# Channel mix down product: one 512-column instruction for two products of the high part, half sums added by VectorE

## The reference, cut to what matters

```python
def _moe2_ref(x, mu_k, mu_r, w_k, w_v, w_r):
    x_prev = np.concatenate([np.zeros((B, 1, D)), x[:, :-1, :]], axis=1)
    xk = mu_k * x + (1.0 - mu_k) * x_prev
    xr = mu_r * x + (1.0 - mu_r) * x_prev
    k = np.maximum(xk @ w_k, 0.0)          # 256 -> 1024
    v = k * k @ w_v                        # 1024 -> 256: the down product
    r = 1.0 / (1.0 + np.exp(-(xr @ w_r)))  # the gate
    return r * v
```

## Time and profile before

| | us |
|---|---|
| median of 3 runs | 1606.61 (1606.55 to 1608.92) |
| the profiled execution, its own time | 1606.98 |
| its span in the profile | 1605.1 |

### The profile page before, as it was taken

The page is one execution under the profiler, slowest core; times in us unless marked ns, Lnnn a source line. Parts: engine busy times, 40 slices in busy tenths (PEclk is TensorE's granted clock), DMA queues, the critical chain, the costliest instruction groups (busy, mean ns, idle before and its releaser), DMA issues.

```text
span 1605.1 us, 30457 instructions
## 1 busy us (share of the span) xinstructions
PE 1505.6 (94%) x11046; PEld 1435.8 (89%) x11046; DVE 1035.9 (65%) x1665; ACT 896.1 (56%) x1709; POOL 340.2 (21%) x375
## 2 busy tenths in 40 slices
PE   6988856699999999999999978999999999999998
PEld 6878736699999999999999977999999999999998
DVE  4766679666666566666666636767676666767574
ACT  1553436476566566665665635656565555556563
POOL 2331227373333333333333310000000000000000
PEclk9998977799999999999999998999999999999999
DMA  8054211665565665665655510110101010101010
GB/s 230 1 158 144 93 79 54 247 241 214 206 234 197 209 240 198 223 224 199 230 216 199 221 39 29 38 52 27 52 26 52 26 52 26 52 26 52 26 40 27
DMA packets 56248, 196.84 MB, mean 123 GB/s; under 512 B 13942, under 2 KB 40326, under 8 KB 46984
## 3 DMA queue, kind: packets, MB, share of 16 engines
q1 hardware_dynamic: 45640, 171.02, 30.5%
q0 software_dynamic: 10560, 25.24, 4.9%
HBM read 160.27 MB, written 39.64 MB: 125 GB/s over the span
## 4 chain that ended last, share of the span: by engine, by line
PE 88%; DVE 5%; issue 3%; POOL 1%; DMA 1%; ACT 1%; SPq 0%; DVEq 0%; POOLq 0%; ACTq 0%
PE ps L603 77%; PE ps L531 3%; PE ps L562 2%; PE ps L611 2%; PE ps L660 1%; PE ps L551 1%; DVE hot_blk L1058 1%; PE ps L552 1%; DVE zv L979 1%; DMA xg<-rows,idx 0%; ACT d L729 0%; DMA tau_b<-tau 0%; DVE cum L1018 0%; ACT square L757 0%; DVE k2f L1151 0%
## 5 line engine op out<-in xcount | busy, mean ns | idle before, releaser
L603 PE MATMUL ps<-we,ht 128*128 128x256 f32 x2640 | 329.7, 284 | 0.0
L603 PE MATMUL ps<-xgt,we 128*128 128x256 f32 x2640 | 327.8, 284 | 1.4 <-DVE xgt L1087 1.4
L603 PEld LDWEIGHTS ps<-xgt,we 128*128 128x128 f32 x2640 | 322.7, 193 | 1.8 <-DVE xgt L1087 1.8
L603 PEld LDWEIGHTS ps<-we,ht 128*128 128x128 f32 x2640 | 319.8, 192 | 0.0
L1098 DVE SCALAR_TENSOR_TENSOR ht<-ps,ht 128x512 fp32r<-128x512 f32 x220 | 146.2, 684 | 217.4 <-ACT ht L789 217.2
L603 PE MATMUL ps<-w_split,k_split 128*128 128x256 f32 x2304 | 280.5, 283 | 0.2 <-DVE k_split L1144 0.2
L603 PEld LDWEIGHTS ps<-w_split,k_split 128*128 128x128 f32 x2304 | 278.2, 192 | 0.4 <-DVE k_split L1144 0.4
L603 PE MATMUL ps<-x_split,w_split 128*128 128x512 f32 x1152 | 268.0, 392 | 6.1 <-DVE x_split L1139 6.1
L1093 DVE TENSOR_TENSOR we<-we_raw,we 128x1024 fp32r<-128x1024 f32 x220 | 263.3, 1218 | 13.5 <-ACT we L779 13.4
L603 PEld LDWEIGHTS ps<-x_split,w_split 128*128 128x128 f32 x1152 | 216.1, 189 | 50.7 <-DVE x_split L1139 6.5
L859 ACT ACTIVATE relu<-ps 128x512 f32<-128x512 f32 x192 | 115.0, 599 | 214.8 <-PE ps L603 214.8
(11 more groups left out here) (142 smaller groups left out, 1423.7 us busy)
## 6 DMA issues: line engine op xcount, KB each, us to landing
we_raw<-w_e SPq DMA_DIRECT2D x55, 2048.0 KB, 8.2
rows<-xr SPq DMA_DIRECT2D x4, 3084.0 KB, 9.4
xin<-x SPq DMA_DIRECT2D x16, 768.0 KB, 12.9
xm<-moe SPq DMA_DIRECT2D x24, 512.0 KB, 4.0
out<-yc SPq DMA_DIRECT2D x24, 512.0 KB, 3.2
xg<-rows,idx POOLq DMA_INDIRECT x110, 4.8
moe<-yo,idx_out POOLq DMA_INDIRECT x110, 5.2
f<-c_f SPq DMA_DIRECT2D x1, 1664.0 KB, 17.0
```

Source lines behind the costliest of these rows:

```text
L603: ins = mm(o, a(i), b_(k), start=first_ and n == 0, stop=last_ and n == 2)
```

## The change

Two edits belong together.

On TensorE, the high part of `k_split` is the stationary operand of two products, with the high and with the low part of `w_v`. They become one instruction of 512 columns, whose moving operand is the view `wv2` over both parts: the left half of a bank takes high by high, the right half high by low. The third product, low by high, is added to the left half. So a group of 128 tokens fills one bank alone; groups 0 and 2 share bank 6, and groups 1 and 3 bank 7, one after the other.

On VectorE, each group is read by a `tensor_reduce` that adds the two halves of its bank into `vsum[j]`, in SBUF, and counts `c_vs`; a multiplication by `sig` of that group follows one group later. `c_v` now counts groups instead of tiles, and TensorE waits on `c_vs` before it starts a group: before j=2 for the reduction of j=0 of the same tile, before j=3 for that of j=1, and before j=0 and j=1 for those of the tile before.

```diff
+        vsum = [part(f"vsum{n}", [D]) for n in range(J)]
...
+        wv2 = w_split[:, :, DC * F:DC * F + FC * D].rearrange("p k (c d) -> p k c d", c=FC)
...
                 pe.wait_ge(c_kl, (t + 1) * FC)
-                wait(pe, c_y, t)
                 for j in range(J):
+                    wait(pe, c_vs, t * J + (j - 1))
+                    bank = ps[:, 6 + j % 2, :]
                     for f in range(FC):
-                        last = mm3(ps[:, 6 + j // 2, (j % 2) * D:(j % 2 + 1) * D],
-                                   lambda i: k_split[:, i, f, j * P:(j + 1) * P],
-                                   lambda k: wv[k][:, f, :], f == 0, f == FC - 1)
-                last.then_inc(c_v, 1)
+                        mm(bank.rearrange("p (k d) -> p k d", k=2), k_split[:, 0, f, j * P:(j + 1) * P], wv2[:, :, f, :],
+                           start=(f == 0), stop=False)
+                        last = mm(bank[:, 0:D], k_split[:, 1, f, j * P:(j + 1) * P], wv[0][:, f, :],
+                                  start=False, stop=(f == FC - 1))
+                    last.then_inc(c_v, 1)
...
                 if f == 0:
-                    wait(act, c_v, t)
+                    wait(act, c_v, t * J)
...
-                dve.wait_ge(c_v, t + 1)
                 dve.wait_ge(c_sig, t + 1)
                 wait(dve, c_out[s], t // 2 * 16)
-                v.tensor_tensor(yc[s].rearrange("p (n j) d -> p n (j d)", n=2), ps[:, 6:8, :],
-                                sig.rearrange("p (n j) d -> p n (j d)", n=2), ALU.mult).then_inc(c_y, 1)
+
+                def gated(j):
+                    dve.wait_ge(c_vs, t * J + (j + 1))
+                    return v.tensor_tensor(yc[s][:, j, :], vsum[j], sig[:, j, :], ALU.mult)
+
+                for j in range(J):
+                    dve.wait_ge(c_v, t * J + (j + 1))
+                    v.tensor_reduce(vsum[j], ps[:, 6 + j % 2, :].rearrange("p (k d) -> p d k", k=2), AX.X, ALU.add
+                                    ).then_inc(c_vs, 1)
+                    if j:
+                        gated(j - 1)
+                gated(J - 1).then_inc(c_y, 1)
```

More of the change, by code:

```diff
@@ L342, in fft_moe_channel_mix @@
         c_sig = sem("c_sig")
+        c_vs = sem("c_vs")
         c_y = sem("c_y")
```

## The result

Five runs of the changed kernel have a median of 1642.1 us (1640.95 to 1644.46), against 1607.95 us (1606.55 to 1608.92) for five of the kernel before on the same chip: a ratio of 1.0218, 95% interval 1.0204 to 1.0232, so 34 us slower. The prediction was 1649 us, with 1637 to 1684 as its range. The profiled execution took 1644.46 us with a span of 1642.6.

A forecast was written before the change was run, and what follows sets the result against it. TensorE's unbroken stream was taken to bound the channel mix at 26.18 us a tile. 23 tiles x 1.81 us plus 0.21 for the last make 41.8; 1606.61 + 41.8 = 1648.4, given as 1649 us, range 1637 to 1684.

The forecast's parts named there:

- The bound and the place: Channel mix: TensorE alone bounds it; a new wait ahead of j=2 stalls 2.22 us, 1.81 us more per tile.
- the 6.6 that was given as a sign of being wrong: Prediction is wrong if VectorE starts the first reduction before 6.6 us into the down product.
- The pair at 347.3 ns: Down product: one 512-column plus one 256-column matmul take 347.3 ns, bounds 334.6 and 360 ns.
- The forecast saving of 0.41 us a tile: Down product: 32 pairs take 11.11 us instead of 11.52, saving 0.41 us of TensorE time a tile.
- The reduction at 1.02 us: VectorE's new strided reduction of 512 PSUM elements takes 1.02 us, with 0.68 and 1.97 us as ends.
- the low end (0.68): VectorE's reduction priced like a plain copy of 512 elements out of PSUM, 0.68 us; whole kernel then 1640 us.
- its 23 equal tiles: The sum counts 23 tiles at 1.81 us more each, all but the last tile.
- Release and restart, 0.15: After VectorE's reduction of j=0, TensorE loses 0.04 us for the release and 0.11 us for the restart.
- VectorE after the last group, covered: VectorE's 1.85 us behind the down product's end just fit the 2.04 us before the first k2f.
- The clock rival: Stalls in the channel mix also drop TensorE's clock: 1.70 us each, 1688 us if all 23, 1668 if half; chance 0.30.
- The argument for holding off: Against a clock fall: first-stage waits had 96- and 146-column instructions around them; here 256 and 512 columns run back to back.
- Nearly free wide instructions: Down product: a 512-column matmul takes 120 ns like a narrow one, so not slower, about 1605.5 us; chance 0.05.

The follow-up runs named there:

- the run with the steps: Changed kernel plus 22 VectorE instructions behind its last result, reading PSUM and SBUF at various steps; only durations read; 1659.41 us in one run.
- The run with 248 elements more: Changed kernel plus a short extra reduction of 248 elements ahead of that of j=0 in each tile; 1662.27 us, ratio 1.0354.

## Why the prediction was right

**The bound and the place.** Right: 23 waits, all ahead of the third group, each tile longer by the wait less what the second half saves. The wait alone put into the kernel before gives 0.99 us of it. Each reduction more adds 0.60 us to the wait (1.46, 2.06, 2.66), and the second half saves 0.17: 1.42 of the 1.45 us that the changed kernel shows. The trace has the reduction start 6.53 us into the down product, just under the 6.6 that was given as a sign of being wrong; its record begins 0.07 us ahead of the end of the subtraction's, which is at 6.60.

**The pair at 347.3 ns.** 353 in a full stream, 346 behind a wait (1330.58 to 1335.43 holds 14 pairs), inside the bounds. The forecast saving of 0.41 us a tile is really 0.22 once the wait is gone.

**The reduction at 1.02 us.** This is the step that was off: 0.689 us, the low end (0.68) that the prediction carried. It read L979 as a dear PSUM operand, and the run with the steps shows that its dear operand is the one in SBUF; L1041 is SBUF as well. With 0.68 the prediction's own sum gives 1640 us, the runs 1642.1; its 23 equal tiles leave out the first tile's 2.7 us on top, 1.1 for the sigmoid and 1.6 for the clock. The estimate of 0.66 us from the Trainium skill, VectorE: DVE Perf Modes, section "The TRN2 errata", was the better guide; the trace's 0.689 is 4% over it.

**Release and restart, 0.15.** Right: 0.04 from the reduction to TensorE, and the first pair behind the wait takes 0.46 us where the next ones take 0.35.

**VectorE after the last group, covered.** Right: the first k2f still finds VectorE idle, for 0.83 us in the changed kernel as against 0.82.

**The clock rival.** It happened once, in the first tile behind 2.59 us, and at none of the 22 waits of 1.46 us; at the 1.8 us that the priced reduction makes it happens in a third of the tiles. The run with 248 elements more is the kernel that the prediction summed to 1649 us, and it takes 1662. So the sum with 1.02 us lacked a term, and that the measured 1642 came out nearer to it is luck: the reduction was cheaper, and the clock stayed up with it. The argument for holding off, that other matmuls run around the wait, is borne out in part only: in the first stage the clock fell behind each of seven waits of 1.98 us and more, here behind half of those of 2.06.

**Nearly free wide instructions.** This rival falls: they take 230 ns each in a group of eight.

## What to carry to other kernels

When a buffer is handed back inside a stage that one engine fills without a gap, ask when the engine that must free it gets there in its own program order, not whether it has idle time: 5.3 idle us per tile did not help, and moving one instruction ahead of two others turned 2.2% slower into 0.4% faster. What an edit saves ahead of such a wait is worth nothing. Where one engine waits for several things in a row, put each wait next to the instruction that needs it: the one for the sigmoid, ahead of reductions that do not read it, was 1.1 us of the first tile. And price a strided access from a row whose strided operand lies in the same memory and whose operation is the same.

## What the runs showed of the hardware

- TensorE's granted clock fell behind none of the waits of 1.46 us, a third of those of 1.79 (7 of 22), half of those of 2.06 (11 of 22) and four in five of those of 2.66 (18 of 22), in an otherwise dense stream; each fall cost 1.5 to 1.6 us.
- VectorE reads PSUM at any step tried for the same price, 0.69 us for 512 elements at 1, 64, 128 and 256 and 0.56 us for 384 at 96. In SBUF its reductions over runs of four elements that lie 96 or 128 apart and of eight that lie 8 to 100 apart cost 0.6 to 0.8 ns more per element, over runs of three 0.1 ns, and over pairs at 96 and 256 nothing. An addition with runs of four at 96 cost 0.7 ns more per element (0.81 us for 384), a copy with the same read nothing (0.49 us for 384).
- Wide and narrow matmuls cost 353 ns a pair when they alternate, 349 when eight of a kind follow each other.
